# Moving one weight load, five information scatters and one register load in a fused attention and expert kernel

## The reference

```python
scores = scale * np.matmul(x, state.transpose(0, 1, 3, 2))
a = softmax(scores);   xread = np.matmul(a, state)
scores2 = scale * np.matmul(state, x.transpose(0, 1, 3, 2))
a2 = softmax(scores2); sread = np.matmul(a2, x)
out = np.concatenate([xread, sread], axis=2)
```

## Time and profile before

| | |
|---|---|
| three runs | 1362.22, 1363.97, 1364.86 us |
| the profiled execution's own time | 1362.22 us |
| its span, first to last instruction | 1360.4 us |
| granted TensorE clock, mean | 0.997 |
| PE busy | 1332.1 us (98%) |
| DVE, ACT, POOL busy | 775.4, 406.9, 386.6 us |
| attention steps on PE | 14 to 142 us |
| experts on PE | 155 to 600 us |
| dense layer on PE | 586 us to the end |

### The profile page before, as it was taken

One profiled execution on the slowest core, in us unless ns is written; L12 is line 12 of the kernel. 1 busy time (PEld: TensorE's weight loads), 2 busy tenths in 40 slices (PEclk: granted clock), 3 DMA queues, 4 the chain that ended last, 5 costly groups with the idle time before them and its releaser, 6 DMA issues.

```text
span 1360.4 us, 19969 instructions
## 1 busy us (share of the span) xinstructions
PE 1332.1 (98%) x6638; PEld 1115.1 (82%) x6639; DVE 775.4 (57%) x1518; ACT 406.9 (30%) x640; POOL 386.6 (28%) x213
## 2 busy tenths in 40 slices
PE   8999899999999999999999999999999999999996
PEld 6998788888888888888888888888888888888885
DVE  4666788888888888854444444444444444444342
ACT  3564222222222222322222222222222222222232
POOL 2377580966590939370010100100001001010010
PEclk9999999999999999999999999999999999999998
DMA  6556341443442425520010100100100001010000
GB/s 141 170 167 198 124 165 52 140 137 129 148 139 77 139 92 187 163 94 16 16 39 16 39 16 16 40 16 9 47 16 33 18 13 40 16 37 2 1 32 16
DMA packets 80460, 100.57 MB, mean 74 GB/s; under 512 B 46096, under 2 KB 46096, under 8 KB 79888
## 3 DMA queue, kind: packets, MB, share of 16 engines
q1 hardware_dynamic: 60016, 61.68, 15.0%
q10 hardware_dynamic: 13856, 20.19, 4.9%
q0 software_dynamic: 6528, 17.87, 3.5%
HBM read 69.80 MB, written 29.92 MB: 73 GB/s over the span
## 4 chain that ended last, share of the span: by engine, by line
PE 94%; DVE 2%; DMA 1%; issue 1%; ACT 1%; ACTq 0%; SPq 0%; POOL 0%; POOLq 0%; DVEq 0%
PE area L1653 27%; PE area L1667 27%; PE area L1599 15%; PE area L1585 15%; PE area L1382 2%; PE area L1352 2%; PE area L1559 1%; PE area L1639 1%; PE area L1372 1%; DMA stage<-in_moe_w 1%; PE area L1339 1%; PE area L1406 0%; PE area L1399 0%; DMA st_diag<-in_state 0%; SPq L334 0%
## 5 line engine op out<-in xcount | busy, mean ns | idle before, releaser
L1667 PE MATMUL area<-W,gs 128*128 128x512 f32 x1632 | 397.7, 392 | 1.0 <-DVE gs L1246 1.0
L1653 PE MATMUL area<-ys,W 128*128 128x512 f32 (+1 forms) x1728 | 394.4, 377 | 0.0
L1653 PEld LDWEIGHTS area<-ys,W 128*128 128x128 f32 x1728 | 313.4, 188 | 61.2
L1667 PEld LDWEIGHTS area<-W,gs 128*128 128x128 f32 x1632 | 303.0, 188 | 63.0 <-DVE gs L1246 1.4
L1193 DVE STREAM_TRANSPOSE area<-hrow 32x256 f32<-32x256 f32 x592 | 269.9, 456 | 77.4 <-ACT hrow L720 68.4
L604 POOL DMA_INDIRECT out<-orow,out_row x34 | 32.7, 961 | 708.7 <-ACT orow L799 701.1
L783 ACT ACTIVATE gate<-gate,half_col 128x512 f32<-128x512 f32 (+1 forms) x144 | 100.7, 699 | 441.0 <-DVE gate L1241 439.9
L1241 DVE TENSOR_SCALAR gate<-area 128x512 f32<-128x512 f32 (+1 forms) x144 | 95.3, 662 | 224.6 <-PE area L1653 224.5
L1599 PE MATMUL area<-W,hs 128*128 x912 | 217.5, 394 | 0.0
L1585 PE MATMUL area<-W,xs 128*128 x888 | 208.1, 390 | 3.5 <-issue 3.5
L1585 PEld LDWEIGHTS area<-W,xs 128*128 128x128 f32 x888 | 166.4, 188 | 38.2 <-issue 3.7
(11 more groups left out here) (184 smaller groups left out, 786.0 us busy)
## 6 DMA issues: line engine op xcount, KB each, us to landing
stage<-in_moe_w SPq DMA_DIRECT2D x32, 1024.0 KB, 5.4
sorted_y<-ytile ACTq DMA_DIRECT2D x38, 256.0 KB, 2.1
xtile<-slot_x ACTq DMA_DIRECT2D x36, 256.0 KB, 2.7
yrow<-sorted_y SPq DMA_DIRECT2D x34, 256.0 KB, 2.7
xin<-in_x SPq DMA_DIRECT2D x60, 128.0 KB, 3.0
stage<-in_moe_w_in SPq DMA_DIRECT2D x4, 1024.0 KB, 4.9
stage<-in_moe_w_out SPq DMA_DIRECT2D x4, 1024.0 KB, 5.8
slot_x<-zero SPq DMA_DIRECT2D x8, 256.0 KB, 3.2
```

Source lines behind the costliest of these rows:

```text
L1653: last = nc.tensor.matmul(HIDDEN[n % 2][:, 0:width], wq[:, wp, :], ys[par][:, yp, k, 0:width], start=(k == 0 and wp == HI and yp == HI), s ...
L1667: last = nc.tensor.matmul(SUMS[a], gs[n % 2][:, gp, a * P:(a + 1) * P], W[:, q // 2 + 2, wp, at:at + DM], start=(n == 0 and gp == HI and w ...
```

## The change

It has three edits. The load of expert 0's unit 2 goes from behind batch 5's `x` to behind batch 4's. Each `scatter_info` comes one expert later, so that expert 1's split has none and that of `w_in` (which runs as expert 8) has the last four. PE's register load of `tail` goes behind the first loop of turns, and `down(0)` goes ahead of the wait for `tables_done`.

```diff
                 if b == 2:
                     for q in range(2):
                         load_unit(expert_unit(0, q), q)
-                if b in (B - 3, B - 2):
-                    q = 2 if b == B - 3 else 3
+                if b in (B - 4, B - 2):
+                    q = 2 if b == B - 4 else 3
                     sp.wait_ge(weights_split, q - 1)
                     load_unit(expert_unit(0, q), q % 2)
@@
             pool.sem_inc(scatter_go, 1)
+            for q in range(4):
+                split_unit(1, q, 4 + q)
 
             def scatter_info(e):
-                for t in range((e - 1) * 5, min(e * 5, TT)):
+                for t in range((e - 2) * 5, min((e - 1) * 5, TT)):
                     pool.indirect_dma_start(out=sorted_info[:, :],
                                             out_offset=bass.IndirectOffsetOnAxis(ap=row_slot[:, t:t + 1], axis=0),
                                             in_=info[:, t, :], in_offset=None).then_inc(info_scattered, 16)
-
-            for q in range(4):
-                split_unit(1, q, 4 + q)
-                if q == 1:
-                    scatter_info(1)
@@
             turn_x(2)
-            pe.wait_ge(tables_done, 5)
-            tail = pe.value_load(settled[0:1, 0:1], min_val=TT - 3, max_val=TILES - 3)
             down(0, True)
@@
+            pe.wait_ge(tables_done, 5)
             with pe.Fori(2, TT - 2) as t:
                 turn(t)
+            tail = pe.value_load(settled[0:1, 0:1], min_val=TT - 3, max_val=TILES - 3)
             with pe.Fori(TT - 2, TILES - 2) as t:
                 with pe.If(t < tail + 1):
                     turn(t)
```

## The result

| | before | after |
|---|---|---|
| median of 15 runs each | 1364.81 us (1362.22 to 1365.83) | 1372.60 us (1366.68 to 1375.10) |
| profiled execution, its own time | 1362.22 us | 1372.05 us |
| its span | 1360.4 us | 1370.3 us |
| granted clock, mean | 0.997 | 0.993 |

The ratio is 1.0051, with a 95% interval of 1.0042 to 1.0060: the change makes the kernel 7.0 us (5.7 to 8.2) slower. (The ratio takes in 22 runs of the new kernel; the medians of the table are 7.8 us apart.) The prediction said slower, at 1368.2 us with 1371.5 as its upper end. The direction is right, the size is too small, and the time lies outside the range. Of the 4.4 us between forecast and measured time, 0.8 us is the kernel before itself: its median of three runs, to which the forecast was added, was 1363.97 us, and of 15 it is 1364.81.

A forecast was written before the change was run, and what follows sets the result against it. PE, holding 94% of the chain that ended last, was taken to bound the kernel. Attention's 4.2 us, 0 for the scatters and 0 for the register load, added to the median of 1363.97, made 1368.2 us; range 1364.6 to 1371.5.

The forecast's parts named there:

- It is worth 0 to PE: Attention, step 5: removing ACT's 2.87 us wait for unit 2 gains PE 0, as line 1406 had no wait.
- The faster rival: Attention, step 6: PE's 1.67 us wait for unit 3 goes, giving 1363.4 us or 1362.3; chance 0.06.
- The price in attention: Unit 2 ahead of batch 5's loads delays batch 5: 3.7 us plus 0.5 for POOL's scatters, 4.2 us; bounds 1.1 to 6.3.
- the second half as deciding: Batch 5 in attention: halves late by 3.45 and 3.66 us count as one delay, the larger, 3.7 us.
- With 3 us ... the list is complete at 552 us.: Before the dense layer: last list scatter, issued at 549.0 us, lands after 3 us, taken from an undisturbed load's 2.9.
- the cover of 1 us: Dense layer's start: ACT weighs the second tile by 561.0 us, PE transposes the first at 561.97, so lateness costs 0.
- The upper end of 2.5: Dense layer's start: PE waits 2.5 us if the last list scatter lands after 6.5 us.
- The clock: Attention: PE's clock falls in the new gap of about 4 us, costing 2.4 us more, 1370.6 us; chance 0.12.
- one stretch of 3.50 us: PE's longest idle stretch, before line 1585, had granted clock 1.00 behind it; said not to decide on a slightly longer one.
- the late list: Dense layer's start: the list of rows is late, PE waits up to 2.5 us in addition, 1370.7 us; chance 0.07.
- Register load: PE's load of `tail`, 0.32 us: moving it gains and costs 0; without cover, under 0.7 us in all.

The follow-up runs named there:

- third edit alone: Only the register load of `tail` moved behind the first loop of turns, against the kernel before: ratio 0.9999 (0.9986 to 1.0011).
- second edit alone: Only the row list's scatters come one expert later, against the kernel before: ratio 1.0023 (1.0009 to 1.0038), 3.1 us.
- the filled ones: Kernel before plus 24 constant transposes in routing's idle stretch: 0.9987; also 8 wide matmuls at the start: 0.9992; also ACT's cast behind its copies: 0.9982.
- the first and the second edit alone: Against the kernel before: only unit 2's load moved ahead of batch 5, 1.0020 (1.0007 to 1.0032); only the list's scatters one expert later, 1.0023.
- late list with tiles first: List's scatters one expert later, SP issuing the first two tiles of `y` ahead of the list, against the kernel before: 1.0027 (1.0016 to 1.0038).

## Why the prediction was wrong, step by step

**"It is worth 0 to PE" (unit 2's late landing).** It holds for the profiled pair. It isn't general: in the profiles of the second and the third edit alone, where unit 2 stands where it did, the same line of step 5 waits 0.51 and 1.64 us. The row of the third:

```profile
98.48 1.09 PE L1406 MATMUL area<-ident,prob 128*128 128x128 f32 x8 [1.64 <-ACT prob L640]
```

Unit 2 landed 7.1 us after its issue in before's profile and 9.3 us in this one. The edit therefore can save up to 1.6 us in some runs. That may be one reason why alone it costs 2.7 us in the ratio and more in its profile, where step 5's first transposes of `prob` start 4.7 us later than in the profile of the second edit alone (98.67 for 93.99) and step 6's first transposes of `x` 4.0 us later (106.91 for 102.91); how often a run has that wait isn't known. The faster rival's sign, step 6's missing wait of 1.67 us, was seen in the changed kernel, but also where nothing near it was changed (the second edit alone): it comes and goes between runs.

**The price in attention.** SP's issue (80.27 for 80.42) and the order of the queue came as predicted, and the first half landed at 88.05 us for 88.3. PE's transposes of it, at 85.08 in before, started at 88.09: 3.0 us later, of which 0.5 was there already, from a late copy of `xT` on DVE, so the edit's own gap is 2.5 us. The sum took the second half as deciding, at 3.7 us. It had no idle time ahead; but the matmuls between the halves were slow, 4.4 us from half to half where before had 2.7 (85.08 to 87.74), so at full clock it might have been late. The sum's 4.2 us for this edit stands against 2.7 (1.0 to 4.4) measured: inside the interval, and rather too much than too little. In the profiled pair 3.0 us of it are left at 147 us. That the sum comes near is in part luck, as it had neither the clock's fall (1.8 us) nor the vanished wait for unit 3 (1.67 us), which work against each other.

**"With 3 us ... the list is complete at 552 us."** This is the step that failed: the landing of the last scatter, put at 3 us, took 7.7, and the cover of 1 us was taken to hide it. The last scatter's issue was right: 554.37 us is the 549.0 of the sum plus the 5.4 us by which PE, for which POOL waits, was late by then. Its landing had no row, and the sum took the 2.9 us of an `x` load. In the four profiles with a late list 6.8 to 8.1 us pass from the last issue to SP's load of the list. The sum goes on as it was: 4.7 us more for the landing, 1.6 less because list and tiles were at ACT 6.7 us behind the issue of the list and not 8.3, and 1.0 of cover gone make 2.1 us; PE's idle time is 2.3. The upper end of 2.5 held for this idle time, but the rival had 0.07, and a wait for the list came in each of the four. Alone the edit costs 3.1 us (1.2 to 5.2) where the sum had 0, and the forecast lacks 2.8, 7.0 against 4.2. With the last four scatters ahead of `w_in`'s split it costs 0 again (0.9999).

**The clock.** It was a rival at 0.12, argued down by one stretch of 3.50 us that passed without a fall. That stretch is the exception. The same place has a lower clock in the stretch 155 to 170 us in every later profile but the filled ones:

```profile
155.00:170.00 15.00, 10.15 (x40) 7.71 (x39) 13.00 (x48) 3.13 (x6) 5.04 (x6) 0.89 0.41 139
```

This is the third edit alone, unchanged there; the first and the second edit alone have 0.77. Behind the new gaps of 2.3 to 3.8 us the clock fell in each profile; behind the one of 1.37 us, in the late list with tiles first, it didn't. Its price, by groups at both clocks: in attention (1.42 - 1.04) + (2.02 - 1.08) + (1.53 - 1.04) = 1.8 us, with 1.08 from before's row of the same four matmuls; at the dense layer 6.66 - 5.75 = 0.9 us, against the `up` of the late list with tiles first. The transposes of `y` ahead of it, 1.73 us for 1.03, add nothing: the 1.85 us from them to `up` pass at the upper clock as well, for the second tile. Before's row:

```profile
85.95 1.08 PE L1372 MATMUL area<-st_diag,pT 128*128 x4
```

The Trainium skill (TensorE: Matmul & The Clock Gate, part on the HAM clock gate) has the clock halve after idle time and return after a busy stretch; the rows agree with both (0.53 from 88.90 to 92.30 us, and the eight transposes at 92.49 at their full speed of 1.04 us). The 1.8 and 0.9 us measured are below the 2.4 us that I took for one fall.

**The range.** The clock and the late list were priced as alternatives to each other and to the forecast. They follow from one another: in each profile with one of the longer gaps the clock's fall came with it. 4.2 us, 2.5 for the list and one fall of 2.4 make 9.1 us, and the range left this out on purpose. **Register load**: 0, as predicted.

**What the profiled pair adds.** The 9.9 us are 3.0 from attention, 2.4 from routing and 4.4 from the dense layer's start. No edit touches routing: 0.8 us there are longer waits, and 1.6 the clock's fall (the first `up` to the second takes 4.8 us for 3.2), which before's profiled run was spared. Its other runs have no profile, but the ten other profiles without filling there all show the fall.

## What to carry to other kernels

A term without a row needs a bound from the least favourable kind of transfer, and a cover of 1 us is no cover against it; ask for each moved transfer who waits for its landing, not only for its issue. Count an idle stretch of PE like these of 2.3 to 3.8 us twice, for itself and for the 0.9 to 1.8 us that the lower clock behind it cost here, and where there are two such stretches add them: cases that can happen together are no alternatives. A wait that one profile shows at 0, or a stretch that it passes at full clock, may be that run's luck, above all if the profiled run is the fastest.

## What was not expected of the hardware

- The last of four scatters of 128 rows of 8 bytes lands 6.8 to 8.1 us after its issue (by the time at which SP, which waits for it, goes on), later than scatters of 2 KB rows (5.0 to 6.5). Why is open.
- In attention 1 MB weight loads land after 5.4 us (unit 2 moved ahead) to 9.6 us (unit 3, third edit alone). What shares the DMA engines with them differs; which transfer decides was not tried.
- Matmuls whose result nobody reads, in a gap that is there anyway, saved 1.8 us (ratio 0.9987, 0.9978 to 0.9996). The clock stayed at 1.00 behind them in all three profiles with this filling, and was 0.77 to 0.89 (155 to 170 us) in ten of the eleven without it.
- DVE's copies of `xT` hold PE up by 0.2 to 0.5 us in one or two steps of some runs, and in three to six steps, 1.7 to 2.9 us in all, in the four profiles of the round with the slowest kernel before. The trace names only a remote cause; it stays open.
